# Rounds two and three of a dense layer as seven 256-token block products per step

## What is computed

```
def _moe2_ref(x, w_gate, w_val, w_out, rms_g):     # x 1536x512, w_gate and w_val 512x1536, w_out 1536x512
    rms = np.sqrt(np.mean(x * x, axis=-1, keepdims=True) + 1e-06)
    xn = x / rms * rms_g
    g = xn @ w_gate
    silu = g * (1.0 / (1.0 + np.exp(-g)))
    val = xn @ w_val
    return (silu * val @ w_out).astype(np.float32)
```

## Time and profile before

| | us |
|---|---|
| median of 3 runs | 720.84 |
| the profiled execution | 721.32 |
| its span, first to last instruction | 719.5 |
| of it before the dense layer's first step (gate of step 0 starts) | 429.1 |
| the 36 steps, up to the start of the outputs left over | 277.0 |
| TensorE busy in the span | 642.2 (89%) |
| mean granted TensorE clock | 0.958 of full speed |

### The profile page before, as it was taken

The page is one execution under the profiler, slowest core; times in us unless marked ns, Lnnn a source line. Parts: engine busy times, 40 slices in busy tenths (PEclk is TensorE's granted clock), DMA queues, the critical chain, the costliest instruction groups (busy, mean ns, idle before and its releaser), DMA issues.

```text
span 719.5 us, 14747 instructions
## 1 busy us (share of the span) xinstructions
PE 642.2 (89%) x6238; PEld 416.1 (58%) x6274; DVE 364.3 (51%) x644; ACT 292.8 (41%) x498; POOL 406.2 (56%) x246
## 2 busy tenths in 40 slices
PE   3799999999997019999999889999999999999997
PEld 1256666666675029999998874444444444444442
DVE  6878888988973805444556545232222223222321
ACT  1355655655654007675667744231121111121112
POOL 5377777877876499798979954652222111131112
PEclk9999999999999559999999679999999999999999
DMA  6986495584494277777778890000000000010001
GB/s 175 236 210 125 129 217 112 144 206 103 107 341 182 100 193 180 257 288 243 264 245 303 304 374 8 1 0 1 1 21 38 1 0 1 1 58 1 1 0 59
DMA packets 59282, 94.11 MB, mean 131 GB/s; under 512 B 30192, under 2 KB 34416, under 8 KB 58192
## 3 DMA queue, kind: packets, MB, share of 16 engines
q1 hardware_dynamic: 57296, 86.86, 41.2%
q0 software_dynamic: 1920, 6.31, 2.3%
HBM read 76.72 MB, written 6.30 MB: 115 GB/s over the span
## 4 chain that ended last, share of the span: by engine, by line
PE 76%; DVE 13%; DMA 3%; issue 3%; ACT 2%; POOL 2%; SPq 1%; POOLq 0%; DVEq 0%; ACTq 0%
PE psum L778 9%; PE psum L779 9%; PE psum L777 9%; PE psum L787 4%; PE psum L788 4%; PE psum L789 4%; PE psum L576 3%; PE psum L733 3%; PE psum L735 3%; PE psum L734 3%; PE psum L714 3%; PE psum L715 3%; PE psum L716 3%; PE psum L590 3%; DVE psum L1050 3%
## 5 line engine op out<-in xcount | busy, mean ns | idle before, releaser
L1376 POOL TENSOR_TENSOR s_lo<-sv,s_hi 128x512 bf16<-128x512 f32 x36 | 41.5, 1153 | 197.4 <-ACT s_hi L833 197.1
L1301 POOL TENSOR_TENSOR probs_lo<-probs 128x768 bf16<-128x768 f32 x80 | 118.5, 1490 | 60.0 <-ACT probs L871 59.7
L1330 POOL TENSOR_TENSOR low<-ring 128x4096 bf16<-128x4096 f32 x20 | 139.9, 7013 | 15.6 <-DMA ring<-in_moe_w 15.6
L871 ACT ACTIVATE probs<-psum 128x384 f32<-128x384 f32 x192 | 92.4, 489 | 72.0 <-PE psum L591 69.3
L778 PE MATMUL psum<-y,ring 128*128 128x512 bf16 x284 | 107.6, 379 | 0.4
L779 PE MATMUL psum<-y,low 128*128 128x512 bf16 x282 | 106.9, 379 | 0.2
L777 PE MATMUL psum<-y,ring 128*128 128x512 bf16 x280 | 106.1, 379 | 0.3
L1258 DVE TENSOR_TENSOR gp<-psum,inv_at 128x512 f32<-128x512 f32 x36 | 24.9, 691 | 150.1 <-PE psum L779 146.3
L1050 DVE TENSOR_REDUCE psum<-psum 128x1 f32<-128x768 f32 x96 | 88.5, 960 | 15.2 <-PE psum L576 14.5
L966 ACT ACTIVATE sig<-gp 128x512 f32<-128x512 f32 x36 | 22.7, 630 | 138.1 <-DVE gp L1258 138.1
L1214 DVE SCALAR_TENSOR_TENSOR hT<-psum,hT 128x512 bf16<-128x512 f32 x80 | 53.9, 689 | 38.6 <-ACT hT L890 37.4
(11 more groups left out here) (194 smaller groups left out, 1456.3 us busy)
## 6 DMA issues: line engine op xcount, KB each, us to landing
ring<-in_moe_w SPq DMA_DIRECT2D x20, 2048.0 KB, 8.6
pair_in<-in_qk SPq DMA_DIRECT2D x8, 1152.0 KB, 5.8
head<-in_qk SPq DMA_DIRECT2D x16, 384.0 KB
head<-in_qk SPq DMA_DIRECT2D x32, 192.0 KB, 5.4
head<-pair_in SPq DMA_DIRECT2D x32, 192.0 KB, 3.6
value<-in_v SPq DMA_DIRECT2D x16, 192.0 KB, 5.9
ring<-in_moe_w_gate SPq DMA_DIRECT2D x4, 768.0 KB, 9.5
ring<-in_moe_w_val SPq DMA_DIRECT2D x4, 768.0 KB, 11.0
```

What stands on the lines that cost most here:

```text
L871: nc.scalar.activation(probs[h % 2][:, t, half * HALF:(half + 1) * HALF], bank(ST_BANK + n % 2)[:, 0:HALF], ACT.Exp, scale=SCALE).then_inc ...
L1301: G.tensor_tensor(probs_lo[par][:, t, :], probs[par][:, t, :], probs_up[par][:, t, :], ALU.subtract)\
L1330: G.tensor_tensor(low[k % RING][:, :], ring[k % RING][:, :], upper[k % RING][:, :, 1], ALU.subtract)\
```

## The change

In rounds two and three (steps 12 to 35) gate and value come from seven products of blocks instead of eight (Strassen's method in Winograd's form). The three things that are halved: the 512-wide contraction (planes 0, 1 and planes 2, 3), the output (gate and value), and the 512 tokens of a round (two halves of 256). A block product contracts 256 rows into 128 x 256 results, so it is 2 planes x 3 matmuls of 256 columns.

The operands are sums:

- per piece f, in round one: sums of gate and value weights (`mix_weights(f)`): VectorE forms them in fp32 into one buffer, `mix` (512 + 512 + 256 elements a partition), ScalarE copies their high parts (1024, then 256 elements), GpSimd makes the low parts (1024, then 256). They overwrite what round one needs no longer. This stands at the end of step n = f + 1.
- per round: sums of tokens, already multiplied by `inv_at` (`mix_columns(i)`): four quarters for round two at steps 7, 8, 9, 10 and four for round three at steps 14, 16, 18, 20 (`COLUMN_AT`). VectorE forms them in five instructions (512, 512, 128, 256, 256), ScalarE copies the high parts (1024), GpSimd makes the low parts (1024).

There is one `mix` buffer: VectorE starts a job only when GpSimd has done the low parts of the job before (`mix_low`).

The 7 products go to banks 0 to 3, which no longer alternate (`seven_blocks`). ScalarE copies the parts that are used twice or first (`copy_blocks`: 512, 256, 256 elements), VectorE adds the others in (`join_blocks`: 512, 256, 512, 256, 512 elements), which gives gate and value side by side in SBUF; then Silu and the product with the value, then s_hi and s_lo as before. In all 36 steps ScalarE's Silu takes the place of the sigmoid and VectorE's product gp x sig is gone. The outputs of rounds two and three are copied without a scale. TensorE does project(10) before the first `seven_blocks`. At the end tile 2 of steps 33 and 34 is done before the last wait.

The diff, cut to what matters:

```diff
+COLUMN_AT = [7, 8, 9, 10, 14, 16, 18, 20]
+READY, COPIES, TAKES = 4, 3, 5
+def job_of_weights(f):
+    return f + sum(n <= f for n in COLUMN_AT)
+def job_of_columns(i):
+    return i + min(COLUMN_AT[i], KF2)
...
 # TensorE
+            def block(o, jj, high, low_part, c, operand, first, last):
+                x_hi, x_lo = (columns_of(c, jj, part)[:, operand // 2, operand % 2, :] for part in range(2))
+                mm(o, high, x_hi, start=first, stop=False)
+                mm(o, high, x_lo, start=False, stop=False)
+                return mm(o, low_part, x_hi, start=False, stop=last)
...
+            def seven_blocks(n):
+                c, f, m = n // KF2, n % KF2, n - KF2
+                if c == 1:
+                    pe.wait_ge(mix_low, job_of_weights(f) + 1)
+                if f == 0:
+                    pe.wait_ge(mix_low, job_of_columns(4 * c - 1) + 1)
+                left, right = slice(0, SUB), slice(SUB, GROUP)
+                if m:
+                    pe.wait_ge(blocks_copied, COPIES * (m - 1) + 1)
+                else:
+                    pe.wait_ge(sv_ready, KF2 - 1)
+                crossed(bank(0)[:, left], c, f, B_CROSS).then_inc(blocks_ready, 1)
+                if m:
+                    pe.wait_ge(blocks_copied, COPIES * (m - 1) + 2)
+                    pe.wait_ge(blocks_taken, TAKES * (m - 1) + 1)
+                plain(bank(1)[:, left], c, f, 1, B_STEP)
+                mixed(bank(1)[:, right], c, f, C_STEP, B_UPPER).then_inc(blocks_ready, 1)
+                if m:
+                    pe.wait_ge(blocks_copied, COPIES * m)
+                    pe.wait_ge(blocks_taken, TAKES * (m - 1) + 3)
+                else:
+                    pe.wait_ge(sv_ready, KF2)
+                mixed(bank(2)[:, left], c, f, C_OWN, B_OTHER)
+                mixed(bank(2)[:, right], c, f, C_VALUE, B_OWN).then_inc(blocks_ready, 1)
+                if m:
+                    pe.wait_ge(blocks_taken, TAKES * m)
+                mixed(bank(3)[:, left], c, f, C_BACK, B_LOWER)
+                plain(bank(3)[:, right], c, f, 0, B_BACK).then_inc(blocks_ready, 1)
...
-            for n in range(2, STEPS):
+            for n in range(2, KF2):
                 gate_and_value(n)
+                project(n - 2)
+            project(KF2 - 2)
+            seven_blocks(KF2)
+            for n in range(KF2 + 1, STEPS):
+                seven_blocks(n)
                 if n < STEPS - 1:
                     project(n - 2)
...
 # ScalarE
+            def copy_blocks(n):
+                m, four = n - KF2, four_of(n)
+                act.wait_ge(slo_ready, n - 1)
+                act.wait_ge(blocks_ready, READY * m + 1)
+                copy(four[:, 1:3, :], bank(0)[:, 0:SUB]....broadcast_to([P, 2, SUB])).then_inc(blocks_copied, 1)
+                act.wait_ge(blocks_ready, READY * m + 2)
+                copy(four[:, 3, :], bank(1)[:, 0:SUB]).then_inc(blocks_copied, 1)
+                act.wait_ge(blocks_ready, READY * m + 3)
+                copy(four[:, 0, :], bank(2)[:, 0:SUB]).then_inc(blocks_copied, 1)
...
             for n in range(STEPS):
-                act.wait_ge(gp_ready, n + 1)
+                if n < KF2:
+                    act.wait_ge(gp_ready, n + 1)
+                else:
+                    copy_blocks(n)
+                    act.wait_ge(blocks_taken, TAKES * (n - KF2 + 1))
                 if n >= 2:
-                    act.wait_ge(silu_ready, n - 1)
-                nc.scalar.activation(sig[n % 2][:, :], gp[n % 2][:, :], ACT.Sigmoid).then_inc(sig_ready, 1)
+                    act.wait_ge(sv_ready, n - 1)
+                nc.scalar.activation(silu[n % 2][:, :], gp[n % 2], ACT.Silu).then_inc(silu_ready, 1)
...
+                if 1 <= n <= KF2:
+                    weights_high(n - 1)
+                if n in COLUMN_AT:
+                    columns_high(COLUMN_AT.index(n))
...
 # VectorE
+            def mix_weights(f):
+                if job_of_weights(f):
+                    dve.wait_ge(mix_low, job_of_weights(f))
...
+            def mix_columns(i):
+                dve.wait_ge(mix_low, job_of_columns(i))
...
+            for n in range(STEPS):
+                if n < KF2:
+                    gate_and_value(n)
+                else:
+                    join_blocks(n)
+                if 1 <= n <= KF2:
+                    mix_weights(n - 1)
+                if n in COLUMN_AT:
+                    mix_columns(COLUMN_AT.index(n))
...
 # GpSimd
             for n in range(STEPS):
                 pool.wait_ge(shi_ready, n + 1)
                 G.tensor_tensor(s_lo[n % 3][:, :], ...).then_inc(slo_ready, 1)
                 if n + OUT_AHEAD < KF2:
                     split_out(n + OUT_AHEAD)
                 if n in SPLIT_AT:
                     split_group(SPLIT_AT.index(n) + 2)
+                if 1 <= n <= KF2:
+                    weights_low(n - 1)
+                if n in COLUMN_AT:
+                    columns_low(COLUMN_AT.index(n))
```

More of the change, by code:

```diff
@@ L54 @@
 OUT_AHEAD = 2
+COLUMN_AT = [7, 8, 9, 10, 14, 16, 18, 20]
+SUB = GROUP // 2
+QUARTER = GROUP // 4
+C_OWN, C_VALUE, C_STEP, C_BACK, C_CROSS = range(5)
+B_OWN, B_OTHER, B_SPARE, B_CROSS, B_BACK, B_STEP, B_UPPER, B_LOWER = range(8)
+READY, COPIES, TAKES = 4, 3, 5
 PENALTY = 2.0 ** 20
@@ L218, in build @@
         unused = sb("unused", [P, TT], F32, at)
+        mix = sb("mix", [P, 5 * 2 * P], F32, at)
         assert at[0] <= nc.sbuf_usable_end, at
@@ L278, in build, with mixed_high, mixed_low, cross @@
         w_low = [group_of(x) for x in low]
+        mixed_rows = [x[:, 0:GWORDS].bitcast(BF16).rearrange("p (r c) -> p r c", r=2 * KD)[:, 2:6, :] for x in ring]
+        low_rows = [x[:, 0:GWORDS].rearrange("p (r c) -> p r c", r=2 * KD) for x in low]
+        def mixed_high(f):
+            g, i = f // GF, f % GF
+            return mixed_rows[g][:, :, i * 2 * P:(i + 1) * 2 * P]
+        def mixed_low(f):
+            g, i = f // GF, f % GF
+            tail = low[g][:, GWORDS:ITEM] if i == 2 else ring[g][:, GWORDS + 512 * i:GWORDS + 512 * (i + 1)].bitcast(BF16)
+            return tail.rearrange("p (r c) -> p r c", r=4)
+        def cross(f, part):
+            g, i = f // GF, f % GF
+            return low_rows[g][:, 2 + 2 * part:4 + 2 * part, i * P:(i + 1) * P]
+        def columns_of(c, jj, part):
+            first = c * GROUP if part else (NTOK if c == 1 else 0)
+            return y[:, :, jj::2, first:first + GROUP].rearrange("p a k c -> p (a k) c")\
+                .rearrange("p m (h c) -> p m h c", h=2)
         psum = ctx.enter_context(nc.psum_tensor("psum", [P, 8, 512], F32))
@@ L782, in gate_and_value, with mixed @@
                         spread(0)
+            def block(o, jj, high, low_part, c, operand, first, last):
[3 more added lines that the diff above has]
+                return mm(o, low_part, x_hi, start=False, stop=last)
+            def mixed(o, c, f, unit, operand):
+                for jj in range(2):
+                    cols = slice(jj * P, (jj + 1) * P)
+                    last = block(o, jj, mixed_high(f)[:, unit, cols], mixed_low(f)[:, unit, cols], c, operand, jj == 0, jj == 1)
+                return last
@@ new lines, in crossed, with plain @@
+            def crossed(o, c, f, operand):
+                for jj in range(2):
+                    last = block(o, jj, cross(f, 0)[:, jj, :], cross(f, 1)[:, jj, :], c, operand, jj == 0, jj == 1)
+                return last
+            def plain(o, c, f, a, operand):
+                g, cols = f // GF, slice((f % GF) * P, (f % GF + 1) * P)
+                for jj in range(2):
+                    j = 2 * a + jj
+                    last = block(o, jj, w_up[g][:, a, j, cols], w_low[g][:, a, j, cols], c, operand, jj == 0, jj == 1)
+                return last
@@ L821, in _ @@
                     project_tile(n, t)
+            for n in (STEPS - 3, STEPS - 2):
+                project_tile(n, 2)
             pe.wait_ge(slo_ready, STEPS)
@@ L824, in _ @@
                 project_tile(STEPS - 1, t)
-            for t in range(2, GT):
-                for n in (STEPS - 3, STEPS - 2, STEPS - 1):
-                    project_tile(n, t)
+            project_tile(STEPS - 1, 2)
+            for n in (STEPS - 3, STEPS - 2, STEPS - 1):
+                project_tile(n, 3)
         @block.scalar
```

109 lines of the change are left out of this document (92 added, 17 removed).

## The result

| | before | after |
|---|---|---|
| median, us (4 runs each) | 720.88 | 738.16 |
| all runs, us | 719.41 to 721.77 | 737.03 to 739.77 |
| profiled execution, us (span) | 721.32 (719.5) | 737.03 (735.2) |
| TensorE busy in the span, us | 642.2 | 635.4 |

The ratio is 1.0234, 95% interval 1.0211 to 1.0256: the changed kernel is 2.3% slower. The prediction said 744 us, 722 to 753, slower with a chance of 0.82.

A forecast was written before the change was run, and what follows sets the result against it. TensorE, busy 89% of the span, was taken to bound the kernel, with the mix jobs binding after the change: 721.3 - 14.3 + 24 + 10.5 + 0.7 + 0.5 + 1 = 744 us, range 722 to 753.

The forecast's parts named there:

- The forecast case: Before step 12, the jobs on the one mix buffer bind; 733 to 752 us, chance 0.56.
- block products: Rounds two and three: 42 matmuls of 256 columns for 24 of 512, 0.109 us each; -14.3 us in 24 steps.
- jobs before step 12: Round one: jobs pass one by one through VectorE, ScalarE, GpSimd, so step 12 starts at 547, not 523; +24 us.
- joins and jobs in rounds two and three: Steps 12 to 35: quarters of tokens, last weights jobs and output copies lengthen the join chain; +10.5 us, bounds 3 and 16.
- end and stores: After the last products: longer final chain to s_lo, +0.7 us, and stores of three tiles in close order, +0.5 us.
- clock: After the last wait before step 12, TensorE runs about 4 us at half clock; +1 us, between 0 and 4.
- The rival without turn-taking: Jobs before step 12: VectorE and GpSimd hardly cut into each other, 10 us late; 724 us, chance 0.17.
- The stated lower bound of 3: Rounds two and three: low end of the +10.5 us, counting only what exceeds the slack once.
- They turn at a step with both of about 10.5 us.: Faster rival's threshold for a step with both job kinds, below which the chain stays hidden; typically 713 us, chance 0.13.
- While the jobs bind, a slow TensorE costs nothing: Before step 12: TensorE at lowered clock after waits of 5 to 8 us adds no time while jobs bind.
- Silu for the sigmoid: All steps, ScalarE: same instruction length, so nothing; if twice 0.63 us, at most a further 4 us from the quarters.

The follow-up runs named there:

- the kernel that takes the turn-taking away: Against the changed kernel, each sum of a job replaced by a same-size VectorE pass over one operand, one buffer kept; 722.63 us.
- the one with both edits: Against the changed kernel, a second buffer for the weights' sums of blocks 0 to 9, and one-operand passes in place of the sums; 708.60 us.

## Why the prediction was right, and where it was off

The forecast case held: direction, mechanism and place. Term by term:

| term | forecast, us | measured, us |
|---|---|---|
| block products | -14.3 | -14.3 (0.109 a matmul) |
| jobs before step 12 | +24 | +24.8 (26.2 counted from step 3's start) |
| joins and jobs in rounds two and three | **+10.5** | **about +2.6** |
| end and stores | +1.2 | +0.8 |
| clock | +1 | +1.7 |
| time | 744 | 738.2 (profiled 737.0) |

- *Products.* A line through 128 and 512 columns gave 256 exactly. The weight load of 98 ns stays hidden behind 109 ns. The Trainium skill, "TensorE: Matmul & The Clock Gate", section "Back-to-back issue gap", gives sustained figures for streams with weight loads by which, as the prediction estimated, there would be no gain; the step of 7.25 us settles that against them.
- *Jobs.* Intervals 7.69, 11.6 and 13.4 us for the forecast 7.5, 11.4 and 13.0; first block matmul at 547.97 for 547; the four waits 4.05, 4.05, 6.08 and 6.44 for 4, 5, 7.5 and 7.5, shorter because the matmuls behind them ran at half clock. That 547.97 is so close to 547 is in part luck: the first job began at 441.19 instead of 443, and 1.4 us of this is the early start of the whole layer, which nobody had forecast; against it, the jobs were longer than forecast, since GpSimd's 1024 elements cost 2.13 us where the line from the earlier trace rows gave 1.9. ScalarE's prices of 1.05 and 0.4 us for 1024 and 256 elements came true (1.06 and 0.40), but not from the rows named: a line through 0.63 and 0.49 gives 1.19 and 0.35. The rival without turn-taking fell with sums of 1.6 us; and the kernel that takes the turn-taking away came to 722.6 where that rival's working had 724.
- *Joins: the term that was mis-sized.* "Joining is a chain too: copies 0.63 + 0.40 ..., 6.1 us", and then 3.9 us more per quarter against 14.5 us for two steps. I added up durations. In the trace instructions that follow each other on VectorE start 0.61 and 0.33 us apart, for durations of 0.69 and 0.42. The closed chain measured 5.45 us, not 6.1. A quarter puts 3.6 us into it, not 3.9: behind the one of step 14 ScalarE starts the copies at 577.50, where 573.9 would have been their turn behind `s_hi`. Two steps with a quarter thus need 2 x 5.45 + 3.6 = 14.5 us, just what TensorE needs, instead of the forecast 16.1, and that is why the quarters of steps 16, 18 and 20 cost nothing. Only the quarter of step 14 shows, with 1.19 and 0.25 us before the products of step 16. It comes behind the last weights job and round one's four output copies without a plain step between: first joins start at 552.72, 561.63, 569.40, 578.45 and 583.91, and ScalarE's copies before the last four of them wait for no matmul. All single waits of rounds two and three, which the prediction had at 6.4 and 4 us, come to 2.1. The stated lower bound of 3 ("only what exceeds the slack once") was the right reading.
- *"They turn at a step with both of about 10.5 us."* The kernel with two buffers has 11.3 us and is slower than before, the one with both edits keeps TensorE's pace of 7.8 and is faster; nothing was measured between.
- *Clock.* 1.7 us lost behind the last wait, none in the kernel without jobs: a consequence of the waits, as said. "While the jobs bind, a slow TensorE costs nothing" holds for the change and for the kernel with early quarters: from 445 us up to their first joins no row of another engine names TensorE as what it waited for.
- *The end.* Its 0.7 does not follow from its terms: 4.6 - 2.9 - 1.3 is 0.4. From the first to the last of the matmuls left over it is 8.46 us for 8.07, also 0.4; the stores have the other 0.4 for the forecast 0.5.
- *Silu for the sigmoid* cost nothing: 0.61 to 0.63 us.

## What to carry to other kernels

Fewer TensorE columns pay only if what prepares them fits beside TensorE step by step: compare the chain's length in the fullest step with TensorE's step (or over two steps, where a plain one follows: 14.5 us were hidden here), not the engines' busy shares, which were 47 to 63% here. Work that has slack is free and work that has none is paid in full, so doing half of a transformation (the round whose preparation has two rounds of time) can beat doing all of it. Add up chains from start to start, as the timeline shows them, and not from durations.
